# Starting the first two MLP blocks early, in a pause of the matrix engine

## The reference, cut to what matters

```python
def _attn_ref(r, k, v, w, u):
    for t in range(S):
        cur = np.einsum('bhd,bhe->bhde', u[None] * kt, vt)
        y[:, :, t] = np.einsum('bhd,bhde->bhe', rt, state + cur)
        state = wt[:, :, :, None] * state + np.einsum('bhd,bhe->bhde', kt, vt)

def _moe_ref(x, w_in, w_out):
    h = np.maximum(x @ w_in, 0.0)
    return (h * h @ w_out).astype(np.float32)

def _moe2_ref(x, w_skip, w_gate, w1, w2):
    ...
    for e in range(E):
        h = np.maximum(xc[mask] @ w1[e], 0.0)
        y[mask] = gate_w[mask, None] * (h @ w2[e])
```

## Time and profile before

| | |
|---|---|
| median of 3 runs | 773.7 us (772.95 to 773.81) |
| profiled execution | 774.66 us, its span 773.1 us |
| PE busy | 744.8 us, 96% of the span |
| DVE, ACT, POOL busy | 61%, 39%, 30% |
| mean granted TensorE clock | 0.988 of full speed |

### The profile page before, as it was taken

One profiled execution on the slowest core, in us unless ns is written; L12 is line 12 of the kernel. 1 busy time (PEld: TensorE's weight loads), 2 busy tenths in 40 slices (PEclk: granted clock), 3 DMA queues, 4 the chain that ended last, 5 costly groups with the idle time before them and its releaser, 6 DMA issues.

```text
span 773.1 us, 15447 instructions
## 1 busy us (share of the span) xinstructions
PE 744.8 (96%) x5786; PEld 666.4 (86%) x5786; DVE 472.9 (61%) x767; ACT 304.9 (39%) x601; POOL 229.5 (30%) x213
## 2 busy tenths in 40 slices
PE   6799999999999999999999999999999999999695
PEld 3588888888988888888888889999999999998594
DVE  8887877866676676766476645444552336555571
ACT  3555544433333344343343333352241225245441
POOL 8754423222242221511142220254341112213111
PEclk9899999999999999999999999999999999999898
DMA  9886223421132223322231105056455226626600
GB/s 235 246 254 184 73 65 87 120 61 38 42 112 71 62 62 104 94 62 63 71 103 48 40 33 204 34 163 204 153 179 212 64 70 216 214 78 203 213 18 16
DMA packets 51073, 88.35 MB, mean 114 GB/s; under 512 B 6668, under 2 KB 34424, under 8 KB 50992
## 3 DMA queue, kind: packets, MB, share of 16 engines
q1 hardware_dynamic: 42240, 61.21, 28.4%
q0 software_dynamic: 7648, 24.51, 9.0%
q10 hardware_dynamic: 1104, 1.57, 0.6%
HBM read 72.79 MB, written 16.95 MB: 116 GB/s over the span
## 4 chain that ended last, share of the span: by engine, by line
PE 90%; DVE 4%; issue 2%; ACT 2%; DVEq 1%; DMA 0%; SPq 0%; POOL 0%; POOLq 0%; ACTq 0%
PE bank L637 27%; PE bank L639 25%; PE bank L638 25%; PE bank L689 3%; PE bank L718 2%; PE bank L734 2%; PE bank L764 1%; PE bank L698 1%; ACT spare L1028 1%; PE bank L857 1%; PE bank L866 1%; PE bank L723 1%; DVE spare L1279 1%; PE bank L728 1%; DMA work<-sorted_rows 0%
## 5 line engine op out<-in xcount | busy, mean ns | idle before, releaser
L637 PE MATMUL bank<-wo_hi,h_hi 128*128 128x394 f32 (+1 forms) x536 | 187.5, 350 | 0.4 <-issue 0.4
L637 PE MATMUL bank<-xt_hi,wi_hi 128*128 128x512 f32 (+1 forms) x528 | 184.6, 350 | 0.1
L639 PE MATMUL bank<-wo_hi,h_lo 128*128 128x394 f32 (+1 forms) x536 | 182.6, 341 | 0.0
L638 PE MATMUL bank<-wo_lo,h_hi 128*128 128x394 f32 (+1 forms) x536 | 182.2, 340 | 0.0
L639 PE MATMUL bank<-xt_hi,wi_lo 128*128 128x512 f32 (+1 forms) x528 | 180.8, 342 | 0.0
L638 PE MATMUL bank<-xt_lo,wi_hi 128*128 128x512 f32 (+1 forms) x528 | 180.6, 342 | 0.0
L1442 DVE SCALAR_TENSOR_TENSOR hid<-bank,hid 128x512 f32<-128x512 f32 x96 | 65.2, 679 | 133.4 <-ACT hid L1066 133.4
L1066 ACT ACTIVATE hid<-bank 128x512 f32<-128x512 f32 x96 | 57.1, 595 | 158.9 <-PE bank L639 158.8
L1702 POOL TENSOR_TENSOR work<-work 112x512 f32<-112x512 f32 x24 | 35.7, 1486 | 254.4 <-DVE work L1257 250.8
L639 PEld LDWEIGHTS bank<-xt_hi,wi_lo 128*128 128x128 f32 x528 | 100.1, 190 | 12.3
L637 PEld LDWEIGHTS bank<-xt_hi,wi_hi 128*128 128x128 f32 x528 | 100.1, 190 | 11.8 <-issue 1.9
(11 more groups left out here) (170 smaller groups left out, 1020.8 us busy)
## 6 DMA issues: line engine op xcount, KB each, us to landing
work<-rkw SPq DMA_DIRECT2D x48, 192.0 KB, 4.1
spare<-rk_rows SPq DMA_DIRECT2D x22, 384.0 KB, 4.5
work<-sorted_rows SPq DMA_DIRECT2D x24, 193.0 KB
work<-rkw SPq DMA_DIRECT2D x48, 96.0 KB, 3.5
work<-v_rows SPq DMA_DIRECT2D x24, 192.0 KB, 4.1
work<-w POOLq DMA_DIRECT2D x6, 768.0 KB, 5.5
x<-w POOLq DMA_DIRECT2D x6, 768.0 KB, 7.5
out<-x SPq DMA_DIRECT2D x20, 192.0 KB, 2.4
```

Source lines behind the costliest of these rows:

```text
L637: pe.matmul(ps, a_hi, b_hi, start=start, stop=False, skip_group_check=True)
L638: pe.matmul(ps, a_hi, b_lo, start=False, stop=False, skip_group_check=True)
L639: return pe.matmul(ps, a_lo, b_hi, start=False, stop=stop, skip_group_check=True)
```

## The change

Four edits; all concern the head and the first two blocks of chunk 0.

1. PE: after `head_scores(0, 3)`, and ahead of `k_transpose(0, 3)`, a new function `layer1_half(f)` is called for f = 0 and 1. It does, for the first 256 of the 512 tokens (units 0 and 1), the two products of three that need only the high part of the weights. `layer1(0, 0, f)` for f < 2 then does the third product for these 256 columns (`wi_lo`) and all three for the other 256.
2. PE: the dummies after `head_scores` of units 0 to 3 are 1, 4, 1 and 0; they were 0, 2, 2 and 0.
3. DVE: the two masks of unit 2 stand between the reciprocals of unit 3; `decays(1, 0)` goes behind unit 3's masks and `take_xlo(0, 0, 2)`, and `own_term(1, 0)` behind `take_xlo(0, 0, 3)`.
4. POOL: `split_lo(1)` goes ahead of `receptance(1, 0)`.

```diff
@@ layer1
+                cols = slice(f * T, f * T + T)
+                if i == 0 and f < 2:
+                    for k in range(KD):
+                        pe.matmul(HID[f][:, 0:2 * T], wi_lo[:, k, cols], xt_hi[0][:, k, 0:2 * T], start=False,
+                                  stop=(k == KD - 1), skip_group_check=True)
+                tokens = slice(2 * T if i == 0 and f < 2 else 0, B * T)
                 for k in range(KD):
-                    cols = slice(f * T, f * T + T)
-                    last = three(HID[f % 2][:, :], wi_hi[:, k, cols], wi_lo[:, k, cols],
-                                 xt_hi[par][:, k, :], xt_lo[par][:, k, :], k == 0, k == KD - 1)
+                    last = three(HID[f % 2][:, tokens], wi_hi[:, k, cols], wi_lo[:, k, cols],
+                                 xt_hi[par][:, k, tokens], xt_lo[par][:, k, tokens], k == 0, k == KD - 1)
                 last.then_inc(ps_hid, 1)
+
+            def layer1_half(f):
+                pe.wait_ge(w_hi, 1)
+                pe.wait_ge(sb_xlo, 2)
+                cols = slice(f * T, f * T + T)
+                for k in range(KD):
+                    for x in (xt_hi[0], xt_lo[0]):
+                        pe.matmul(HID[f][:, 0:2 * T], wi_hi[:, k, cols], x[:, k, 0:2 * T],
+                                  start=(k == 0 and x is xt_hi[0]), stop=False, skip_group_check=True)
@@ PE, head
                 head_scores(0, b)
-                if b == 1 or b == 2:
-                    keep_busy(2)
+                keep_busy((1, 4, 1, 0)[b])
+                if b == 3:
+                    for f in range(2):
+                        layer1_half(f)
                 k_transpose(0, b)
@@ DVE, head
-            for b in range(2):
-                decays(0, b + 2)
-                inverses(0, b + 2)
-                mask_scores(0, b + 1, 0)
-                mask_scores(0, b + 1, 1)
-                own_term(0, b + 2)
-                take_xlo(0, 0, b)
-            decays(1, 0)
+            decays(0, 2)
+            inverses(0, 2)
+            mask_scores(0, 1, 0)
+            mask_scores(0, 1, 1)
+            own_term(0, 2)
+            take_xlo(0, 0, 0)
+            decays(0, 3)
+            inverse(0, 3, 0)
+            mask_scores(0, 2, 0)
+            mask_scores(0, 2, 1)
+            inverse(0, 3, 1)
+            own_term(0, 3)
+            take_xlo(0, 0, 1)
             split_lo(0)
             mask_scores(0, 3, 0)
             mask_scores(0, 3, 1)
+            take_xlo(0, 0, 2)
+            decays(1, 0)
+            take_xlo(0, 0, 3)
             own_term(1, 0)
-            take_xlo(0, 0, 2)
-            take_xlo(0, 0, 3)
             inverse(1, 0, 0)
@@ POOL, head
             own_rows(1, 0)
+            split_lo(1)
             receptance(1, 0)
-            split_lo(1)
             keys(1, 0)
```

## The result

The changed kernel takes 765.73 us (median of 5, 764.82 to 766.55), the kernel before 773.7 (772.95 to 775.44, 5 runs on the same chip): ratio 0.9894, 95% interval 0.9878 to 0.9910. The profiled execution took 766.55 us, its span is 765.0. Every trace shows one execution, and a mark in it is worth no more than that; medians and ratios are of all executions.

A forecast was written before the change was run, and what follows sets the result against it. PE was taken as the bound behind the head, with mask waits and half clock as the head's losses. Head terms summed to −1.9 us, from a median of 773.7 to 771.8 us; range 771.0 to 773.6.

The forecast's parts named there:

- What the head gives up reaches the end of the kernel unchanged: Behind the head PE is the bound, so the head's gain passes through if nothing PE needs comes late.
- and the same distances from there on: Sign of being right: behind block 2, near 43.6 us, PE's marks keep their spacing.
- the sum: Head to block 2: −1.0, +0.2, −0.85, −0.65, +1.05 and −0.65 us, together −1.9 us.
- My last rival: The head's shift doesn't reach the end, since some expert load sets the same end: 773.7 us, chance 0.02.
- Units 1 and 2, scores of unit 3: Head: full clock after unit 1's shortened pause, 1.26 us; unit 3's scores at 32.5 instead of 33.49, gain 1.0 us.
- Masks of unit 3: Head, DVE: masks start at 34.17 instead of 34.97 and end at 35.53; transposes 0.8 us earlier, at 35.6.
- Early halves: Before unit 3's transposes: twelve 256-column matmuls at 0.12 us, hidden under the masks with 0.2 us of cover.
- Clock of unit 3: Unit 3's transposes to block 0 at full clock: 2.85 us instead of 3.69, block 0 at 38.4.
- The load: Transposed w_out piece for the gate product after block 0: lands at 41.05 after 8.7 us; PE pauses 1.15 us.
- the third rival: The w_out load doesn't move, PE waits 2.4 us and goes to half clock: 774.8 us, chance 0.07.
- The second limit: Chain from block 1's ReLU to piece 2 on POOL, needed by block 4: caps the gain near 2 us.

The follow-up runs named there:

- + 128: Kernel before, with 128 idle semaphore increments on PE spread over the first-layer blocks of chunks 1 to 5: 770.46 us, ratio 0.9941.
- before + 46: Kernel before, with 46 idle semaphore increments on PE, in two placings: ahead of its first wait 769.45 us, spread over chunks 1 to 5 769.06 us.
- after + 210: Changed kernel with 210 idle semaphore increments on PE in chunks 1 to 5, 256 instructions more than the kernel before: 774.33 us, ratio 0.9994.
- after + 24: Changed kernel with 24 idle semaphore increments on PE in chunks 1 to 5, 70 instructions more than the kernel before: 765.83 us, ratio 0.9887.
- before + 46 in the chunks: Kernel before, with 46 idle semaphore increments on PE spread over the first-layer blocks of chunks 1 to 5: 769.06 us, ratio 0.9923.

## Why the prediction was wrong

The thirteen kernels fall in groups by one thing, the length of PE's code ahead of the experts. With 0 or 256 instructions more the experts take 209.2 to 210.4 us, with 38 to 70 more 201.2 to 202.0, with 128 more 203.2, whatever DVE, POOL and the dummies do. The edits' meaning plays no part: increments do it as well, at the start or in the chunks. What is shown is that the stop hangs on where the code lies. That it is the fetch of a jump's target is inferred, from "issue", from the place between two experts' items, and from this: the Trainium skill ("Runtime: NRT & Kernel Launch", section Instruction fetch mechanics) says that instruction memory is refilled in blocks of 16 KiB, 256 instructions, ahead in sequence, and that a taken branch whose target isn't at hand forces a fetch. By that rule, as I read it, a shift by a whole block restores the old placing; here + 256 restored the stop (5.3 us), and + 128 put another in its place. The traces bear it out further. A DMA queue that the profile names "instruction" moves 48 or 49 packets of 16 KB in the whole span. In the three kernels with the long stop one of them starts 2 to 4 us into the stop, and none in the 13 us ahead of it. In the nine without a stop of over 1.2 us that packet starts 7 to 9 us into the item ahead, while PE still has work. Before, from 717.26 to 723.29 (no packet from 706.50 to 717.26):

```profile
q8 instruction: 1, 0.02, 1.1%
```

In + 128 it is less clear: a packet starts just ahead of its stop. Which engine this queue serves isn't shown, so the fetch stays inferred, though well supported.

By the prediction's own steps:

- **"What the head gives up reaches the end of the kernel unchanged"** together with "and the same distances from there on" is the step that failed, and with it the sum, which holds terms of the head only and puts everything behind block 2 at nothing. The head's gain passed on, as said, but the distances did not stay: the sum lacked a term of −7.6 us in the experts, for what 46 more instructions on PE do to the stop. My last rival spoke of later stages, and only of giving back. It could have been read: I asked for PE's waits up to 45 us. Over the whole span the largest is "issue", 7.4 us, and the diff adds instructions ahead of it. That wouldn't have told the sign of a new placing, but it would have put the low end near 764.
- **Units 1 and 2, scores of unit 3**: right. Full clock from 24.10, scores at 32.86 for a forecast of 32.9 with unit 0's drift. But the 1.26 us that I credited to the clock are those of one execution: after the same pause ahead of unit 1 (2.61 and 2.62 us) the clock stayed 1.00 in both kernels before + 46. So this gain hung on the execution that was profiled.
- **Masks of unit 3**: 0.7 us late. I let `split_lo(0)` wait for the keys alone (from 32.0 to 34.16, 2.2 us, and four traces show 2.24 to 2.27), but here POOL's next product went ahead of it. I had seen that the two exclude each other and stopped at one product.
- **Early halves**: right, 1.41 us from the first start to the last for twelve times 0.12, hidden; 1.1 us of cover instead of 0.2, because the masks were late.
- **Clock of unit 3**: right: from the transposes to block 0 2.90 us for 2.85, at 1.00.
- **The load**: it was issued at 32.79 and PE's weight load for it came at 41.88, 9.1 us later (8.9 before), where I had 8.8; PE waited 0.6 us instead of 1.15, since it was late itself. Once, in after + 210, the third rival's mechanism showed: a wait of 2.3 us there, and a head of 556.17.
- **The second limit**: it capped the gain at 0.74 us, not near 2. I let ACT's ReLU follow the gate product by 3.38 us; it follows DVE's row, which is as long as before and began with the same reciprocal at 39.85. I had not priced `own_term` on DVE, which edit 3 put between the last `take_xlo` and that reciprocal: 0.46 us, as much as `take_xlo` gained.

What the head is worth is less sure than what the experts are. The profiled executions give 0.55 us, 0.89 in after + 24 and 0.81 for the DVE and POOL edits alone. The medians allow more: the change stands at 0.9894 and before + 46 in the chunks, with the old head, at 0.9923, a difference of 2.2 us between intervals that just overlap. That would be as much as the 1.9 that I forecast, but the chain to block 4, by which I had it, gave 0.7 to 1.1 us: what speaks for more is the steadier clock of the new dummies over all executions.

Open: the length at which the stop sets in between 70, 128 and 256, the early halves' own worth, and how the head's gain divides between clock and order.

## What to carry to other kernels

Read the waits of the bottleneck engine over the whole span before you price an edit, also where the edit is far away: a wait for "issue" of some microseconds at a loop's or an expert's jump is an amount that a change of the code's length ahead of it may win or lose. Before you credit a change with a gain, pad the old kernel with as many idle instructions as the change added (not at its very start, where 46 of them cost 3.5 us here), and see what is left. Compare the medians for that and not one trace: a trace can be of the fastest execution. When two engines shut each other out, ask what follows on the other engine: here a waiting instruction was held through two of its instructions in four traces and through one in four.

## What the runs showed of the hardware

- A stop of 5.3 to 6.2 us at one jump of PE's code, with the granted clock at 0.83 or 0.84 in the 20 us around its end, present or not by the code's length: with 38 to 70 instructions more it was gone (0.8 to 1.2 us at a later jump are there in before, too), with 128 more it was 2.7 us one jump earlier, with 256 more it was back.
- 46 semaphore increments ahead of PE's first matmul moved it from 4.16 to 8.23 us. Without them PE waited for DVE until 4.16, so they took between 4.1 and 8.2 us. Spread over the chunks they cost nothing that shows: from block 4 to the first expert pair are 499.27 us before, 499.30 with 46 and 499.21 with 210.
- A DVE operation of 1.74 us with two inputs in SBUF was held through POOL's keys and the product behind them in four traces (3.20 or 3.21 us), and through the keys alone in four (2.24 to 2.27).
- Pauses of PE of 2.60 to 2.63 us in the head: after that of unit 1 the granted clock fell to 0.50 in before, and stayed 1.00 in both kernels before + 46.
